# A gated linear attention with two mixture layers: exponents in one product, P kept in PSUM, the causal mask on POOL

## The reference

```
m_new  = max(f_t + m, i_t)
C = exp(f_t + m - m_new) * C + exp(i_t - m_new) * outer(v_t, k_t)
n = exp(f_t + m - m_new) * n + exp(i_t - m_new) * k_t
y_t = sigmoid(o_t) * (C q_t) / max(|n . q_t|, 1)
```

## Time and profile before

| | |
|---|---|
| median of the runs | 331.17 us |
| profiled execution | 331.48 us |
| its span | 329.3 us |
| TensorE busy | 276.9 us (84%) |
| VectorE busy | 256.8 us (78%) |
| POOL busy | 174.3 us (53%) |
| ACT busy | 144.4 us (44%) |

### The profile page before, as it was taken

How to read it: one execution, slowest core, us unless ns; L and a number is a source line. 1 busy time by engine, 2 the same in 40 slices (tenths; PEclk the granted TensorE clock), 3 DMA queues, 4 the chain that set the end, 5 groups by cost and what they waited for, 6 DMA issues and landing times. The chain is left out here.

```text
span 329.3 us, 8741 instructions
## 1 busy us (share of the span) xinstructions
PE 276.9 (84%) x3311; PEld 202.9 (62%) x3345; DVE 256.8 (78%) x419; ACT 144.4 (44%) x222; POOL 174.3 (53%) x334
## 2 busy tenths in 40 slices
PE   0028999999999999999984898487499999999996
PEld 0025788888888888888872325131166666666664
DVE  8964669999999999998754459213999999999951
ACT  1453012232323222232321073401998888888850
POOL 3602245655556465554540029410688888888880
PEclk9999999999999999999995699989789999999999
DMA  7960038767766865744004999600379999998993
GB/s 236 352 239 0 2 83 282 224 198 262 263 187 206 291 238 170 265 128 116 2 2 145 349 407 430 266 2 0 76 148 171 197 170 212 156 211 189 179 209 106
DMA packets 64553, 60.68 MB, mean 184 GB/s; under 512 B 52800, under 2 KB 56896, under 8 KB 61952
## 3 DMA queue, kind: packets, MB, share of 16 engines
q1 hardware_dynamic: 64512, 60.12, 64.4%
HBM read 43.59 MB, written 3.93 MB: 144 GB/s over the span
## 5 line engine op out<-in xcount | busy, mean ns | idle before, releaser
L904 DVE TENSOR_TENSOR arena<-arena 128x512 bf16<-128x512 f32 x48 | 64.9, 1351 | 0.0
L797 ACT ACTIVATE arena<-ps 128x512 f32<-128x512 f32 x48 | 28.7, 598 | 68.1 <-PE ps L546 68.1
L774 PE MATMUL ps<-wouth,ring 128*128 128x320 bf16 x192 | 54.3, 306 | 1.4 <-DMA ring<-ring 0.9
L775 PE MATMUL ps<-woutl,ring 128*128 128x320 bf16 x192 | 54.2, 305 | 0.0
L896 DVE TENSOR_TENSOR arena<-ps,arena 128x512 f32<-128x512 f32 x48 | 32.9, 686 | 10.9 <-ACT arena L797 8.2
L434 POOL TENSOR_TENSOR arena<-arena 128x328 f32<-128x328 f32 x20 | 15.0, 751 | 45.9 <-ACT arena L797 45.9
L1125 DVE TENSOR_REDUCE ring<-ps 128x1 f32<-128x1024 f32 x24 | 29.2, 1222 | 5.6 <-PE ps L765 5.4
L879 ACT ACTIVATE ring<-ring 128x1024 bf16<-128x1024 f32 x24 | 27.6, 1149 | 10.4 <-POOL ring L527 10.4
L560 PE MATMUL ps<-arena 40*128 40x128 f32 x384 | 30.6, 304 | 1.7 <-DVE arena L896 1.7
L778 PE MATMUL ps<-wouth,ring 128*128 128x320 bf16 x192 | 30.0, 299 | 0.0
L543 PE MATMUL ps<-causal,identb 128*128 128x512 bf16 x25 | 10.6, 424 | 22.3 <-DVE arena L1006 22.3
(11 more groups left out here) (174 smaller groups left out, 689.9 us busy)
## 6 DMA issues: line engine op xcount, KB each, us to landing
ring<-w_dram SPq DMA_DIRECT2D x10, 1280.0 KB, 8.9
arena<-kv_dram SPq DMA_DIRECT2D x24, 324.0 KB, 4.6
arena<-qkT_dram SPq DMA_DIRECT2D x48, 160.0 KB
sig<-o_gate_dram SPq DMA_DIRECT2D x3, 1280.0 KB, 11.4
arena<-w_dram SPq DMA_DIRECT2D x3, 1280.0 KB, 8.8
sig<-w_dram SPq DMA_DIRECT2D x3, 1280.0 KB, 9.6
out_dram<-ring SPq DMA_DIRECT2D x24, 160.0 KB, 2.2
arena<-w_out_dram SPq DMA_DIRECT2D x1, 1280.0 KB, 6.2
```

The source lines that it names most:

```text
L774: pe.matmul(o, UHT[i % 4][:, j, :], wouth[:, j, :], start=(j == 0), stop=False)
L775: pe.matmul(o, UHT[i % 4][:, j, :], woutl[:, j, :], start=False, stop=False)
L797: act.activation(WT[i % 2][:, hf * HALF * L:(hf + 1) * HALF * L], bE, ACT.Exp).then_inc(s["w_ready"], 1)
L904: dve.tensor_tensor(low(pf), pf, high(pf), ALU.subtract).then_inc(s["pl_ready"], 1)
```

## The change

One product makes a half tile's exponents. The rows of `pick` grow from 96 to 99, and A3 gets three rows of ones. Into the three new rows of `pick` SP brings, tile by tile, the three parts of l for the 8 heads of the tile. They come from a copy of L3 in HBM that is written once ahead of the loop. The causal product is gone: POOL sets the exponentials of s after t to zero in place (`mask`), two halves a tile, between the exponential and the product. VectorE writes P over the scores in PSUM, ACT rounds it to bf16 (`p_high`, into PH), and VectorE subtracts the two into PL, also bf16. The scores' banks stay taken until both low parts are written.

The order in a step changes on TensorE, ACT, POOL and VectorE, as the ends of the hunks show. `add_to_state` and its waits are as they were, only earlier in the step.

```diff
@@ -43,6 +43,7 @@
     G3 = 3 * BH
+    GL = G3 + 3
     HB = F // 2
@@ -58,9 +59,8 @@
         lam_first = sb("lam_first", [BH, NC, 1], F32)
-        causal = sb("causal", [P, HALF * L], BF16)
         pick_words = sb("pick_words", [P, BH * L // 2], F32)
-        pick = pick_words[:, :].bitcast(BF16).rearrange("p (h t) -> p h t", h=BH)[0:G3]
+        pick = pick_words[:, :].bitcast(BF16).rearrange("p (h t) -> p h t", h=BH)
         lo_rows_g = sb("lo_rows_g", [P, 1], F32)
@@ -104,7 +104,8 @@
         WT = [carve(H * L) for _ in range(2)]
-        PF = [carve(H * L) for _ in range(2)]
+        PH = [carve(H * L, BF16) for _ in range(2)]
+        PL = [carve(H * L, BF16) for _ in range(2)]
         inter = [carve(H * HV) for _ in range(2)]
@@ -326,12 +328,26 @@
             sp.dma_start(gcol[:, :], g_ln).then_inc(s["gcol_in"], 16)
+            def load_row(i):
+                c, b = i // B, i % B
+                sp.dma_start(pick[G3:GL, b * H:(b + 1) * H, :],
+                             kept.rearrange("(r h) t -> r h t", r=3)[:, b * H:(b + 1) * H, c * L:(c + 1) * L]) \
+                    .then_inc(l_in[b], 16)
             load_tile(2)
             load_tile(3)
+            sp.wait_ge(s["l_ready"], 1)
+            sp.dma_start(kept, L3[0:G3, :]).then_inc(s["l_kept"], 16)
+            sp.wait_ge(s["l_kept"], 16)
+            for i in range(B):
+                load_row(i)
 
             sp.wait_ge(s["rows_ready"], 1)
             sp.wait_ge(s["coefs_ready"], 2)
             for i in range(B, NT):
+                sp.wait_ge(s["e_done"], 2 * (i - B) + 2)
+                load_row(i)
                 sp.wait_ge(s["i_done"], i - B + 1)
@@ -379,14 +395,11 @@
             pool.memset(identf[:, :], 0.0).then_inc(s["pool_step"], 1)
-            pool.memset(lo_rows_g[:, :], 0.0)
-            pool.memset(causal[:, :], 0.0).then_inc(s["pool_step"], 1)
+            pool.memset(lo_rows_g[:, :], 0.0).then_inc(s["pool_step"], 1)
             pool.wait_ge(s["pool_step"], 1)
             pool.affine_select(out=identf[:, :], in_=identf[:, :], compare_op=ALU.not_equal, fill=1.0, base=0,
                                pattern=[[-1, P]], channel_multiplier=1).then_inc(s["ident_ready"], 1)
             pool.wait_ge(s["pool_step"], 2)
-            pool.affine_select(out=causal[:, :], in_=causal[:, :], compare_op=ALU.is_ge, fill=-1e30, base=0,
-                               pattern=[[0, HALF], [1, L]], channel_multiplier=-1).then_inc(s["consts_ready"], 1)
             pool.affine_select(out=lo_rows_g[:, :], in_=lo_rows_g[:, :], compare_op=ALU.is_ge, fill=-1.0,
@@ -422,6 +435,16 @@
 
+            def mask(n, hf):
+                i = tile_at(n, 0)
+                if i is None:
+                    return
+                pool.wait_ge(s["exp_ready"], 2 * i + hf + 1)
+                w = heads(WT[i % 2][:, hf * HALF * L:(hf + 1) * HALF * L], L, HALF)
+                pool.affine_select(out=w, in_=w, compare_op=ALU.is_ge, fill=0.0, base=0,
+                                   pattern=[[0, HALF], [1, L]], channel_multiplier=-1).then_inc(s["w_ready"], 1)
             def decay_values(n):
@@ -467,6 +490,8 @@
             def step(n):
+                mask(n, 0)
+                mask(n, 1)
                 decay_values(n)
@@ -539,12 +564,9 @@
                 head = b * H + HALF * hf
-                await_(pe, "w_ready", 2 * i + hf)
-                pe.matmul(bE, identb[:, :], causal[:, :], start=True, stop=False)
-                pe.matmul(bE, A3[0:G3, c * L:(c + 1) * L], pick[:, head:head + HALF, :], start=False, stop=False)
-                for j in range(HALF):
-                    last = pe.matmul(bE[:, j * L:(j + 1) * L], pick[:, head + j, :], L3[0:G3, c * L:(c + 1) * L],
-                                     start=False, stop=(j == HALF - 1))
+                await_(pe, "exp_ready", 2 * i + hf)
+                pe.wait_ge(l_in[b], 16 * (c + 1))
+                last = pe.matmul(bE, A3[0:GL, c * L:(c + 1) * L], pick[0:GL, head:head + HALF, :], start=True, stop=True)
                 last.then_inc(s["e_done"], 1)
@@ -554,7 +576,7 @@
                 pe.wait_ge(qk_in[b], 32 * (i // B + 1))
-                await_(pe, "p_ready", 2 * i)
+                await_(pe, "pl_ready", 2 * i)
                 for j in range(HALF):
@@ -582,8 +604,7 @@
                     vh, vl = high(values_of(b)[:, cols]), VL[b][:, cols]
-                    p = PF[i % 2][:, h * L:(h + 1) * L]
-                    ph, pl = high(p), low(p)
+                    ph, pl = (p[i % 2][:, h * L:(h + 1) * L] for p in (PH, PL))
                     pe.matmul(bO[:, cols], ph, vh, start=True, stop=False)
@@ -597,7 +618,7 @@
                 await_(pe, "lg_ready", i)
-                await_(pe, "state_ready", min(n - 1, NT - B))
+                await_(pe, "state_ready", min(n, NT - B))
                 for kk in range(NP):
@@ -644,17 +665,17 @@
                 exponents(n, 0)
-                scores(n)
-                exponents(n, 1)
                 if n == 0:
                     coefficients()
+                add_to_state(n)
+                transpose_x(n)
+                exponents(n, 1)
+                scores(n)
                 weigh_values(n)
                 logits(n)
-                add_to_state(n)
-                transpose_x(n)
 
             pe.wait_ge(s["ident_copied"], 1)
-            pe.wait_ge(s["consts_ready"], 3)
+            pe.wait_ge(s["consts_ready"], 2)
             pe.wait_ge(s["rows_ready"], 1)
@@ -794,7 +815,7 @@
                 await_(act, "vd_ready", min(i - 1, NT - B))
-                act.activation(WT[i % 2][:, hf * HALF * L:(hf + 1) * HALF * L], bE, ACT.Exp).then_inc(s["w_ready"], 1)
+                act.activation(WT[i % 2][:, hf * HALF * L:(hf + 1) * HALF * L], bE, ACT.Exp).then_inc(s["exp_ready"], 1)
 
@@ -804,10 +825,21 @@
 
+            def p_high(n, hf):
+                i = tile_at(n, 0)
+                if i is None:
+                    return
+                cols = slice(hf * HALF * L, (hf + 1) * HALF * L)
+                act.wait_ge(s["p_ready"], 2 * i + hf + 1)
+                await_(act, "o_done", i - 1)
+                act.copy(PH[i % 2][:, cols], bS[hf]).then_inc(s["ph_ready"], 1)
             def step(n):
                 weights_of(n, 0)
+                copy_xt(n)
                 weights_of(n, 1)
-                copy_xt(n)
+                p_high(n, 0)
+                p_high(n, 1)
 
@@ -892,16 +924,16 @@
                 dve.wait_ge(s["s_done"], i + 1)
-                await_(dve, "o_done", i - 1)
-                dve.tensor_tensor(PF[i % 2][:, cols], bS[hf], WT[i % 2][:, cols], ALU.mult).then_inc(s["p_ready"], 1)
+                dve.tensor_tensor(bS[hf], bS[hf], WT[i % 2][:, cols], ALU.mult).then_inc(s["p_ready"], 1)
 
             def p_low(n, hf):
                 i = tile_at(n, 0)
                 if i is None:
                     return
-                pf = PF[i % 2][:, hf * HALF * L:(hf + 1) * HALF * L]
-                dve.wait_ge(s["p_ready"], 2 * i + hf + 1)
-                dve.tensor_tensor(low(pf), pf, high(pf), ALU.subtract).then_inc(s["pl_ready"], 1)
+                cols = slice(hf * HALF * L, (hf + 1) * HALF * L)
+                dve.wait_ge(s["ph_ready"], 2 * i + hf + 1)
+                await_(dve, "o_done", i - 1)
+                dve.tensor_tensor(PL[i % 2][:, cols], bS[hf], PH[i % 2][:, cols], ALU.subtract).then_inc(s["pl_ready"], 1)
 
@@ -960,6 +992,7 @@
 
+            dve.memset(A3[G3:GL, :], 1.0)
             for ap in num:
@@ -973,7 +1006,7 @@
             dve.wait_ge(s["dve_const"], 2)
-            dve.tensor_copy(pick, again(own_row[:, :], 2, L)).then_inc(s["consts_ready"], 1)
+            dve.tensor_copy(pick[0:G3], again(own_row[:, :], 2, L)).then_inc(s["consts_ready"], 1)
 
@@ -997,7 +1030,7 @@
             dve.tensor_copy(L3[BH:2 * BH, :], high(rest_l))
-            dve.tensor_tensor(L3[2 * BH:3 * BH, :], rest_l, high(rest_l), ALU.subtract)
+            dve.tensor_tensor(L3[2 * BH:3 * BH, :], rest_l, high(rest_l), ALU.subtract).then_inc(s["l_ready"], 1)
             dve.wait_ge(s["im_ready"], 1)
@@ -1021,17 +1054,17 @@
             def step(n):
-                p_product(n, 0)
                 if n == 0:
                     copy_coefficients()
+                add_state(n)
+                p_product(n, 0)
+                p_product(n, 1)
                 scale_inter(n)
                 p_low(n, 0)
-                p_product(n, 1)
+                p_low(n, 1)
                 sum_up(n)
-                p_low(n, 1)
                 denominator(n)
                 invert(n)
-                add_state(n)
                 copy_logits(n)
```

More of the change, by code:

```diff
@@ L12, with mlstm_softmoe_solu @@
 P = 128
-def mlstm_softmoe_solu(nc, qkT, kv1, o_gate, f_gate, i_gate, phi, w1, w2, w_in, w_out, g_ln, out, dims):
+def mlstm_softmoe_solu(nc, kept, qkT, kv1, o_gate, f_gate, i_gate, phi, w1, w2, w_in, w_out, g_ln, out, dims):
     B, H, S, D, E, SLOTS, F = dims
@@ L189, in mlstm_softmoe_solu @@
```

(10 more changed lines are left out.)

## The result

The changed kernel took 388.12 us in the median of four runs (385.51 to 390.57) beside 331.26 us (328.66 to 331.37); ratio 1.174, interval [1.165, 1.183]. Forecast were 335.9 us, with a range up to 385. The time lies outside the range and close to the first rival's 384 us. The profiled execution took 390.57 us, its span 388.8, against 329.3 before. The last copy of logits, which closes the loop, starts at 233.37 us, 57.5 us later than before the change; the stages behind the loop add 2.

A forecast was written before the change was run, and what follows sets the result against it. TensorE was taken to set the 5.74 us step, and after the change a loop through the logits' copy, 6.19 us. On 331.48 us, +7.2 - 2.1 - 1.0 + 0.3 = +4.4 gave 335.9 us; range 328 to 385.

The forecast's parts named there:

- first rival: Attention loop: TensorE stays at, or falls back to, 1.2 GHz; 8.6 us a step, 384 us; chance 0.33.
- this case: Likeliest case, attention loop at 2.4 GHz after the rise: 6.19 us a step, 336 us, own range 331 to 342; chance 0.42.
- rival 1: Same as the first rival: TensorE at 1.2 GHz in the attention loop, 8.6 us a step, 384 us; chance 0.33.
- 0.6 us for the difference: Early loop steps: part of the gain lost because less work is left when the clock rises, +0.6 us.
- four products are worth 0.88 us: Exponents on TensorE: four fewer 512-column products a step at 0.22 us each; its own work falls from 5.74 to 4.86 us.
- The loop through the logits' copy: Steps 5 to 20: state update waits for VectorE's copy of the logits; 6.19 us against 5.74, +7.2 us in all.
- The second loop: Attention step through sum_up, POOL's gate and divide, mask, products and p_low: the step can't come below 5.68 us.
- Prices of product, p_low, mask, rounding: Attention step: product and p_low on VectorE 0.61 us each, POOL's mask 0.64, ACT's rounding 0.60.
- The second rival: POOL's mask costs more in f32: at 1.18 us the loop takes 6.8 us, total 347 us; chance 0.10.
- Fetched rows, 0.3 us: Prologue: first exponent parts go through HBM and back; +0.3 us, bounds 0 and 3; later transfers cost 0.
- rival 3: Attention loop: VectorE passes PSUM operands faster, so the logits' copy is no limit; 5.5 us a step, 324 us; chance 0.12.

The follow-up runs named there:

- e15: Kernel before, plus one TensorE wait in step 12, ahead of the scores, for the previous step's copy of the logits: 385.90 us (1.167).
- e6: Changed kernel, logits moved to the bank of the products with the state, 16 extra 512-column products once at the start of step 4: 381.40 us (1.151).
- e4: Kernel before, old order, one 512-column exponent product a half, leaving out the mask and the l part: 386.56 us (1.167).
- e12: Kernel before with one 512-column product a half (no mask, no l part), as e4, plus the dense start of e8: 311.72 us (0.943).
- e1: Changed kernel plus 16 extra 512-column products of the exponents' operands, once, at the start of step 4: 391.66 us (1.183).
- e2: Changed kernel plus two extra, overwritten 512-column products ahead of each half's exponents in every step: 419.72 us (1.267).
- e14: Changed kernel with a dense start, 83 products while TensorE waits for the first fetched rows and 12 in step 0: 387.09 us (1.169).
- e13: As e10, with the causal product replaced by the changed kernel's select on POOL for every tile: 385.81 us (1.169).
- e10: Kernel before, old order, dense start of e8, l part of the exponents fetched per tile from tile 4 on: 315.94 us (0.957).
- e11: As e10 without the dense start, so the kernel before with only the fetched l part: 319.04 us (0.966).
- e5: Changed kernel, two extra products ahead of each half's exponents, logits moved to the bank of the products with the state: 420.80 us (1.270).
- e16: Kernel before, plus the wait of e15 in each of steps 12 to 19: 385.05 us (1.163).
- e9: Changed kernel, logits in another bank, four extra products a step ahead of the logits: 329.18 to 331.73 us (four executions), 366.28, 392.56, 415.77 to 417.84 (four).
- e3: Kernel before without the causal product, leaving two of three 512-column products a half: 406.92 us in one execution, 319.12 in the other.
- e8: Kernel before plus dense 512-column products, 60 while TensorE waits for the rows and 20 in step 0: 326.13 us (0.988).

## Why the prediction was wrong

The step that failed is the clock. The sum of the forecast takes the loop at the upper level from its rise on and has no term for losing it, and this case was held for likelier than rival 1 (0.42 against 0.33). The runs showed 8.63 us a step in place of 6.19, 57.5 us over the loop. Two parts of the reasoning failed.

*Holding.* The reason given against rival 1 was the earlier trace rows: TensorE kept the level through a stretch with 1.46 of 4.00 us busy. That stretch was cut off too early. In the next one the same trace shows the level lost (TensorE alone, columns as above; the fall lies between two pairs of equal products):

```profile
232.00:236.00 4.00, 1.54 (x4) 0.75 0.23 45
```
```profile
232.79 0.61 PE L765 MATMUL ps<-pick_words,arena 128*128 128x512 bf16 x2 [2.96 <-DVE ring L1133]
235.07 1.03 PE L765 MATMUL ps<-pick_words,arena 128*128 128x512 bf16 x2 [1.67 <-DVE ring L1133]
```

It shows a hold for some us more, not a loop that keeps the level step after step. In the attention loop a single gap of 1.5 us was enough (e15), and so was 0.67 us in three steps running (e6). The prediction had itself computed an idle time of about 1.3 us a step from step 5 on and counted only the 0.45 us by which it lengthens the step.

*Rising.* The sum lets the clock rise in the lighter loop as it did before and allows 0.6 us for the difference. In the profiled execution it never rose, and there was no wait that could have prevented it. e4 does the same in the old order with thinned exponents alone.

Point by point:
- *TensorE bounds the step; four products are worth 0.88 us.* Right: e12 runs at 4.86 us a step.
- *The loop through the logits' copy.* Its place and its releaser were right (e1, e2, e14: 1.55 to 1.72 us of idle at the state update, released by the copy of the logits; about 1.3 were forecast). Its full price, 6.19 us a step at the upper level, was never seen, since the level was lost in the same step.
- *The second loop, 5.68 us.* Right, e6, with POOL's mask as the releaser.
- *Prices of product, p_low, mask, rounding.* Right within 0.02 us of the rows taken, and two products or two p_low in a row take 1.30 and 1.28 us, so the 0.61 us from start to start was right too. The second rival (a dear mask) is out; e13 shows the mask at its right price but in the wrong place.
- *Fetched rows, 0.3 us.* Wrong: the copy through HBM was 8.1 us under way, and 2.45 us of the delay remained. The bound of 3 held. e10 and e11 avoid it by fetching from tile 4 on.
- *Rival 1.* Right in mechanism and nearly in size: 8.6 us a step forecast, 8.63 measured; 384 us forecast, 388.1 measured; about half of the difference is the fetched rows, 2.45 us in place of 0.3. It named a loop that stays at the lower level and one that falls back to it, and both occur. The profiled execution never rises. Of the other three, one (389.62 us) has the same mean granted clock, 0.965, and two (385.51 and 386.62 us) have 0.755 and 0.752, the number of e1, whose trace shows a rise and a fall at the first wait for the logits; for the changed kernel itself this is inferred.
- *The other side (rival 3).* Not tested: in every trace of the new order with the logits' wait the level was lost at that wait or never there.

The Trainium skill, "TensorE: Matmul & The Clock Gate", section "What's actually happening", was named beside this rival: a monitor sets the clock by how busy the engine has recently been. The falls behind a wait agree (e15: 1.50 us). The 40.00 us of 40.00 that e2 was busy at a granted clock of 0.50 do not follow from it, if busy is what the trace counts as busy.

What stays open: what decides a rise. In e2, e5 and e15 TensorE worked without a gap for 50 us and more at the lower level, with three products a half, and the level did not return; in e16 it did, once, after 59 us. The other unaided rises in these traces came by 41 us, ahead of the scores of step 2 (e11, e15), or at 48 to 61 us, in the steps 3 and 4. e15's is a step earlier than that of the kernel before, with the same instructions up to there. e9's profiled execution (415.77 us) never rose; by their times its executions of 366.28 and 392.56 us had the upper level for a part of the loop. Executions of one program differ (e3, e9), and nothing in the traces says beforehand which gets it. What wait is long enough to lose the level is open too: in the attention loop single ones of 0.61 and 0.63 us did not (e8, e10), and single ones of 0.85 us and more were each followed by a fall (e13, e5, e12); but in a later stage of the kernel before, TensorE kept the level after standing idle for 0.98 us (until 221.74) and 1.51 us (until 228.38), so the length of one wait does not decide alone. How much of the 388 us is thinning and how much waits can't be split either: thinning alone costs 55 us in the old order (e4), and so does one wait alone (e15).

A version that beats both kernels came out: e10, the fetched rows alone, in the old order, with a dense start, at 315.94 us, 4.3% under the kernel before.

## What to carry to other kernels

Where TensorE is gapless and its lengths say 2.4 GHz, treat the level as an asset: a reordering that makes it wait even once may double the length of its work from there on, so count the first wait of a microsecond or so as a chance of that, not as its own microsecond. Take work off such an engine only in an order that keeps it fed, and look for the level in instruction lengths, since the granted clock column can read 1.00 from the start at either level. Taking work off can also keep the level from coming at all, without any wait (e4). A dense block in idle time ahead of a loop is cheap, but no guarantee: it helped where no wait of 0.85 us or more followed (e8, e10), and its level was lost before step 2 in e12, e13 and e14.

## What the runs showed of the hardware

- One idle stretch of 1.50 us of TensorE in the attention loop halved its clock for the 12 steps that were left: +55 us (e15). In e16 two such stretches, at 102 and 169 us, each cost the level.
- The same program can come out at 319 or at 407 us (e3), and anywhere between 329 and 418 (e9); the traces of the long executions show no rise, and that it came in the short ones is inferred.
- Work without a wait does not by itself bring the level back: e2 was busy for 40.00 of 40.00 us at a granted clock of 0.50.
- A light loop (one 512-column product a half, 4.86 us a step) kept 2.4 GHz, while heavier ones with a gap lost it (e12 against e5).
- 80 dense products at the start (60 while TensorE waits, 20 in step 0) brought 5 us in the kernel before (e8), and 3 us in the one with fetched rows (e10 against e11).
